# Attention scores of 24 of 32 pair groups as three products of split queries and keys, with two slots for keys, queries and values

## What is computed

```python
scores = scale * np.matmul(q, k.transpose(0, 1, 3, 2))
kth = np.partition(scores, -top_k, axis=-1)[..., -top_k:-top_k + 1]
mask = scores >= kth
scores = np.where(mask, scores, -1000000000.0)
scores = scores - np.max(scores, axis=-1, keepdims=True)
attn = np.exp(scores)
attn = attn / (np.sum(attn, axis=-1, keepdims=True) + 1e-09)
return np.matmul(attn, v).astype(np.float32)
...
h = x @ w_in
g = np.maximum(0.01 * h, h)
return (g @ w_out).astype(np.float32)
...
h = x @ w_in
g = np.where(pos, h, np.where(neg, 0.0, (h + beta) ** 2 / (4.0 * beta)))
return (g @ w_out).astype(np.float32)
```

## Time and profile before

| | |
|---|---|
| median of 3 runs | 1202.42 us (1201.8 to 1202.47) |
| the profiled execution | 1198.35 us |
| its span in the trace | 1196.4 us |
| busy: PE, DVE, ACT, POOL | 1108.2, 924.3, 701.0, 608.7 us |
| DMA queues of SP and ACT, share of 16 engines | 65.5%, 3.9% |

### The profile page before, as it was taken

One profiled execution on the slowest core, in us unless ns is written; L12 is line 12 of the kernel. 1 busy time (PEld: TensorE's weight loads), 2 busy tenths in 40 slices (PEclk: granted clock), 3 DMA queues, 4 the chain that ended last, 5 costly groups with the idle time before them and its releaser, 6 DMA issues.

```text
span 1196.4 us, 21062 instructions
## 1 busy us (share of the span) xinstructions
PE 1108.2 (93%) x7360; PEld 999.2 (84%) x7360; DVE 924.3 (77%) x2088; ACT 701.0 (59%) x1579; POOL 608.7 (51%) x582
## 2 busy tenths in 40 slices
PE   3547998899999999999999989999899999999998
PEld 2335887778989988889987978998789999999998
DVE  7999999989799998998989999969989006300234
ACT  5676878756577765666666756566775424312232
POOL 5676778835366643655536744346644323222222
PEclk9758999989999999999999999999999999999999
DMA  6789997766667787767666756455356677787764
GB/s 228 280 300 342 348 346 285 270 229 206 220 223 233 255 285 257 275 230 258 236 233 211 249 182 222 159 198 175 121 194 217 201 256 250 252 283 251 250 239 150
DMA packets 86792, 287.12 MB, mean 240 GB/s; under 512 B 9632, under 2 KB 13472, under 8 KB 86688
## 3 DMA queue, kind: packets, MB, share of 16 engines
q1 hardware_dynamic: 79200, 270.04, 65.5%
q10 hardware_dynamic: 7488, 15.73, 3.9%
HBM read 247.46 MB, written 38.27 MB: 239 GB/s over the span
## 4 chain that ended last, share of the span: by engine, by line
PE 71%; DVE 19%; POOL 3%; issue 3%; ACT 3%; DMA 1%; POOLq 0%; SPq 0%; ACTq 0%
PE ps_f L812 19%; PE ps_f L820 19%; PE ps_f L813 18%; DVE top L1067 7%; DVE work L1070 7%; PE ps_av L771 6%; PE ps_s L727 3%; PE ps_t L748 2%; DVE drop L1076 2%; PE ps_t L727 2%; DVE part_r L1094 2%; PE ps_t L754 2%; POOL gate L644 1%; POOL drop L630 1%; POOL part_o L650 1%
## 5 line engine op out<-in xcount | busy, mean ns | idle before, releaser
L1067 DVE MAX8 top<-work 128x8 f32<-128x576 f32 x432 | 309.3, 742 | 0.1
L812 PE MATMUL ps_f<-xy,w_ring 128*128 128x384 f32 (+2 forms) x896 | 288.8, 322 | 4.5 <-ACT xy L994 2.5
L820 PE MATMUL ps_f<-gate,w_ring 128*128 128x384 f32 (+2 forms) x896 | 281.3, 314 | 9.5 <-POOL gate L644 9.4
L812 PE MATMUL ps_f<-gate,w_ring 128*128 128x384 f32 (+2 forms) x896 | 286.0, 319 | 1.0 <-ACT part_o L975 0.6
L630 POOL TENSOR_TENSOR drop<-scores,drop 128x576 f32<-128x576 f32 x144 | 207.9, 1444 | 150.1 <-DVE drop L1076 150.1
L820 PE MATMUL ps_f<-xy,w_ring 128*128 128x384 f32 (+2 forms) x896 | 280.8, 313 | 1.8 <-POOL xy L654 1.6
L813 PE MATMUL ps_f<-xy,w_ring 128*128 128x384 f32 (+2 forms) x896 | 280.1, 313 | 0.0
L813 PE MATMUL ps_f<-gate,w_ring 128*128 128x384 f32 (+2 forms) x896 | 280.0, 312 | 0.0
L1070 DVE MATCH_REPLACE8 work<-top,work 128x576 f32<-128x576 f32 x288 | 212.7, 739 | 0.0
L812 PEld LDWEIGHTS ps_f<-xy,w_ring 128*128 128x128 f32 x896 | 169.7, 189 | 20.5 <-issue 9.3
L644 POOL TENSOR_TENSOR gate<-part_r,gate 128x384 fp32r<-128x384 f32 (+2 forms) x112 | 101.5, 909 | 157.4 <-ACT gate L979 157.2
(11 more groups left out here) (83 smaller groups left out, 1822.0 us busy)
## 6 DMA issues: line engine op xcount, KB each, us to landing
w_ring<-w_split SPq DMA_DIRECT2D x412, 512.0 KB, 4.2
w_split<-w_ring SPq DMA_DIRECT2D x36, 512.0 KB, 6.0
raw<-wd SPq DMA_DIRECT2D x64, 256.0 KB, 4.3
w_split<-xy SPq DMA_DIRECT2D x28, 512.0 KB, 3.7
kq<-kqd ACTq DMA_DIRECT2D x12, 576.0 KB, 5.8
v_sb<-vd ACTq DMA_DIRECT2D x12, 320.0 KB, 3.2
out_t<-y_acc ACTq DMA_DIRECT2D x12, 192.0 KB, 3.6
kq<-kqd SPq DMA_DIRECT2D x3, 576.0 KB, 6.7
```

Of the source, the lines that this page charges most:

```text
L812: pe.matmul(out, w[:, 0, m], high, start=first, stop=False)
L820: mm = pe.matmul(out, w[:, 0, m], low, start=False, stop=end)
L1067: dve.max(top[:, t % T_SLOTS, 8 * r:8 * r + 8], source(t, r)).then_inc(dve_step, 1)
```

## The change

**Scores.** For pair groups 8 to 31 (items 20 to 79, 60 of the 80) `kq` is split: ACT copies the loaded queries and keys of the group into `kq_split` high (`high_kq`, one copy of 832 or 960 columns), POOL subtracts for the low part in two halves of 416 or 480 columns (`low_kq`). Both stand three steps before the group's first score, ACT's at the end of the step before. A half of the scores is then three products for each head, float32r each: 12 source instructions an item, one pass each. The first 20 items keep plain float32.

**Mixed items.** They are now written as 128 x 288 products, both heads over 128 stationary columns, where before they were 64 x 64 tiles with a piece of 64 keys apart. For that the host lays out zeros or the first 64 keys again beside queries and keys.

**Loads.** `kq` and `v_sb` have two slots, used by pair group number, and all their loads are issued by SP: 32 groups of keys and queries (the keys of a pair are loaded for both of its groups), 32 of values. SP waits in its own order for the slot: on scores done, on POOL's low part, on values done.

```diff
+KQ_FREE = [score_step(ITEMS[FIRST_OF_GROUP[gp]]) - KQ_AHEAD + 1 if gp >= FIRST_ROUNDED else
+           score_step(ITEMS[LAST_SCORED[gp]]) + 1 for gp in range(GROUPS)]
+KQ_LOAD_AT = {KQ_FREE[gp - KQ_SLOTS]: gp for gp in range(KQ_SLOTS, GROUPS)}
+KQ_LOWERED_AT = {score_step(ITEMS[FIRST_OF_GROUP[gp]]) - KQ_AHEAD: gp for gp in range(FIRST_ROUNDED, GROUPS)}
+V_LOAD_AT = {values_step(gp - V_SLOTS) + 1: gp for gp in range(V_SLOTS, GROUPS)}
...
+            def load_kq(gp):
+                old = gp - KQ_SLOTS
+                if old >= FIRST_ROUNDED:
+                    sp.wait_ge(kq_low_done, 2 * (old - FIRST_ROUNDED + 1))
+                elif old >= 0:
+                    sp.wait_ge(scores_done, 2 * LAST_SCORED[old] + 2)
+                first, end = kq_span(gp)
+                sp.dma_start(kq[:, gp % KQ_SLOTS, first:end], kqd[gp, :, first:end]).then_inc(kq_loaded[gp % KQ_SLOTS], 16)
+            def load_v(gp):
+                if gp >= V_SLOTS:
+                    sp.wait_ge(av_done, gp - V_SLOTS + 1)
...
             for s in range(len(PLAN)):
+                if s in KQ_LOAD_AT:
+                    load_kq(KQ_LOAD_AT[s])
+                if s in V_LOAD_AT:
+                    load_v(V_LOAD_AT[s])
...
+            def low_kq(gp, part):
+                pool.wait_ge(kq_high_done, gp - FIRST_ROUNDED + 1)
+                first, end = kq_parts(gp)[part]
+                slot = kq_split[:, gp % KQ_SLOTS, :, first:end]
+                pool.tensor_tensor(slot[:, 1, :], kq[:, gp % KQ_SLOTS, first:end], slot[:, 0, :].bitcast(F32),
+                                   ALU.subtract).then_inc(kq_low_done, 1)
...
+                if s in KQ_LOWERED_AT:
+                    low_kq(KQ_LOWERED_AT[s], 0)
                 for u in second:
                     event(u)
                 if s in VALUES_AT and s >= READY[0]:
                     low_x(VALUES_AT[s])
                 for u in third:
                     event(u)
+                if s in KQ_LOWERED_AT:
+                    low_kq(KQ_LOWERED_AT[s], 1)
...
+                if it.gp < FIRST_ROUNDED:
+                    exact = kq[:, it.gp % KQ_SLOTS, :]
+                    terms = [(exact, exact)]
+                else:
+                    high, low = kq_split[:, it.gp % KQ_SLOTS, 0, :], kq_split[:, it.gp % KQ_SLOTS, 1, :]
+                    terms = [(high, high), (low, high), (high, low)]
...
+                    even, odd = Q_COLS + j * PART, Q_COLS + j * PART + (REST if it.mixed else 0)
+                    for n, (q, k) in enumerate(terms):
+                        start, stop = n == 0, n == len(terms) - 1
+                        pe.matmul(out[:, 0, 0:PART], q[0:D, rows[0]], k[0:D, even:even + PART], start=start, stop=stop)
+                        mm = pe.matmul(out[:, 1, 0:PART], q[D:P, rows[1]], k[D:P, odd:odd + PART], start=start, stop=stop)
+                    mm.then_inc(scores_done, 1)
...
-                if it.mixed and it.b + 1 < B:
-                    act.dma_start(kq[:, it.pair, :], kqd[(it.b + 1) * PAIRS + it.pair, :, :]).then_inc(kq_loaded[it.pair], 16)
+
+            def high_kq(gp):
+                act.wait_ge(kq_loaded[gp % KQ_SLOTS], 16 * ((gp + 1) // KQ_SLOTS))
+                if gp >= FIRST_ROUNDED + KQ_SLOTS:
+                    act.wait_ge(scores_done, 2 * LAST_SCORED[gp - KQ_SLOTS] + 2)
+                first, end = kq_span(gp)
+                act.activation(kq_split[:, gp % KQ_SLOTS, 0, first:end], kq[:, gp % KQ_SLOTS, first:end], ACT.Copy).then_inc(kq_high_done, 1)
...
-                if gp // PAIRS % 2 and b + 1 < B:
-                    act.dma_start(v_sb[:, pair, :], vd[(b + 1) * PAIRS + pair, :, :]).then_inc(v_loaded[pair], 16)
...
+                if s + 1 in KQ_LOWERED_AT:
+                    high_kq(KQ_LOWERED_AT[s + 1])
```

More of the change, by code:

```diff
@@ L75 @@
 VECTOR_AHEAD = 2
+Q_COLS = 2 * P + REST
+KQ_COLS = Q_COLS + S + REST
+KQ_SLOTS = 2
+V_SLOTS = 2
+KQ_AHEAD = 3
+FIRST_ROUNDED = 8
 S_SLOTS = 4
@@ L425, in sem @@
             return ctx.enter_context(nc.semaphore(name))
[L427 to L428 removed]
+        kq = sb("kq", [P, KQ_SLOTS, KQ_COLS])
+        kq_split = sb("kq_split", [P, KQ_SLOTS, 2, KQ_COLS], F32R)
+        v_sb = sb("v_sb", [P, V_SLOTS, VC])
         scores = sb("scores", [P, S_SLOTS, 2, S])
@@ L461, in build @@
         kq_first = sem("kq_first")
-        kq_loaded = [sem("kq_loaded%d" % p) for p in range(PAIRS)]
-        v_loaded = [sem("v_loaded%d" % p) for p in range(PAIRS)]
+        kq_loaded = [sem("kq_loaded%d" % a) for a in range(KQ_SLOTS)]
+        kq_high_done = sem("kq_high_done")
+        kq_low_done = sem("kq_low_done")
+        v_loaded = [sem("v_loaded%d" % a) for a in range(V_SLOTS)]
         raw_loaded = [sem("raw_loaded%d" % a) for a in range(RAW_SLOTS)]
@@ L716, in score @@
                     pe.wait_ge(kq_first, 32)
-                elif it.rows == 2 or it.rows == 0 and it.gp:
-                    pe.wait_ge(kq_loaded[it.pair], 16 * (it.b + 1))
+                elif it.gp >= FIRST_ROUNDED:
+                    pe.wait_ge(kq_low_done, 2 * (it.gp - FIRST_ROUNDED + 1))
+                elif it.gp and it.n == FIRST_OF_GROUP[it.gp]:
+                    pe.wait_ge(kq_loaded[it.gp % KQ_SLOTS], 16 * ((it.gp + 1) // KQ_SLOTS))
                 need(pe, scores_copied, 2 * it.n)
@@ L721, in score @@
                     need(pe, p_t_copied, ITEMS_OUT[it.n])
-                q, k = kq[:, it.pair, 0:S], kq[:, it.pair, S:2 * S]
-                for j, out in enumerate(score_halves(it)):
[L724 to L736, removed]
-                    pe.matmul(out[0:D, 0, 0:PART], q[0:D, rows], k[0:D, c0:c1],
-                              start=True, stop=True).then_inc(scores_done, 1)
@@ new lines, in score @@
+                if it.gp < FIRST_ROUNDED:
[4 more added lines that the diff above has]
+                    terms = [(high, high), (low, high), (high, low)]
+                first = it.col + Q_COLS - GROUP_WIDTH[it.group]
+                rows = slice(first, first + P), slice(first, first + P)
+                if it.mixed:
+                    rows = rows[0], slice(first + REST - P, first + REST)
@@ L757, in values @@
             def values(gp):
-                b, pair = gp // PAIRS // 2, gp % PAIRS
+                slot = gp % V_SLOTS
                 width = GROUP_WIDTH[gp // PAIRS % 2]
-                pe.wait_ge(v_loaded[pair], 16 * (b + 1))
+                pe.wait_ge(v_loaded[slot], 16 * (gp // V_SLOTS + 1))
                 pe.wait_ge(p_t_copied, ITEM_OF[LAST_OF_GROUP[gp]].n + 1)
@@ L765, in values @@
                         if c < KC:
-                            w = v_sb[:, pair, (a * KC + c) * D:(a * KC + c + 1) * D]
+                            w = v_sb[:, slot, (a * KC + c) * D:(a * KC + c + 1) * D]
                             x = p_t[:, a * KC + c, 0:width]
                         else:
-                            w = v_sb[:, pair, (2 * KC + a) * D:(2 * KC + a + 1) * D]
+                            w = v_sb[:, slot, (2 * KC + a) * D:(2 * KC + a + 1) * D]
                             x = p_rem[:, 0:width]
```

39 lines of the change are left out of this document (22 added, 17 removed).

## The result

The changed kernel takes 1215.25 us (median of 4 runs, 1214.69 to 1216.73) against 1202.11 for the kernel before beside it (4 runs, 1201.74 to 1202.47): ratio 1.0119, 95% interval 1.0104 to 1.0134. It is 1.2% slower. The forecast, 1197.3 us, and its range, 1191 to 1207, both miss it, and the sign is wrong. The profiled execution took 1216.73 us, and that of before lay some 4 us under its kernel's median, so the two spans (1214.9 and 1196.4) differ by 18.5 us and the medians by 13.1.

What follows compares the result with a forecast made beforehand. PE was taken to bound the kernel, except where DVE leads. Saving -8.1, costs +2 and +1 make -5.1: profiled 1198.35 becomes 1193.2, and with the median 4.07 above it, 1197.3 us; range 1191.7 to 1207.

Steps and rivals of the forecast that it cites:

- DVE's own work sets the pace in those steps. I take 0, within 1 us: At the start, moved loads and raw pieces waiting in SP's queue cost nothing, within 1 us to either side.
- a cover for the net's weights: Net weights queued behind SP's key loads: 7.3 us of cover against a wait of at most 6.0, so hidden.
- if the windows before 195 us move: Stated sign that the prediction is wrong: the start, before any changed item is scored, was to stay as it was.
- The added work at the same rate is 1.4 + 0.5 = 2 us: PE's extra waits for POOL's subtractions (1.4) and ACT's copies (0.5), at present waits per busy time: 2 us.
- 1 us for DVE: DVE's find of the dropped slowed by POOL's added work, 0.7 us, with an allowance for the net's square: 1 us.
- 8.1 us: Part of PE's 10.8 us saving on 60 items' scores that reaches the end of the kernel.
- The count by the chain's shares: Items from 195 to 896 us weighted by the net's lines in the chain of waits: 44.8 items at 0.18 us.
- The score block: An item's scores on PE: six float32r pairs, 0.133 us apart, 0.99 us instead of 1.17, saving 0.18 an item.
- (a): PE's score products save nothing, pairs coming every 0.163 us, so only costs stay: 1205 us, chance 0.14.
- (d): The two heads' float32r score products run one behind the other on PE, 37 us more: 1240 us, chance 0.05.
- Rival (c): POOL's first half delays join and low gate, PE losing 1.1 us at half of 24 groups: 1207 us, chance 0.12.
- The signs: Expected in the profile: PE's waits for POOL's gates under 12 us, DVE's for PE's units below 46.8, forecast operation lengths.

Runs made afterwards that it cites:

- e7: Changed kernel with no group split, all scores in plain float32, and SP's key, query and value loads issued last in each step: 1203.42 us.
- e4: e1 with POOL subtracting 16 columns instead of 416 or 480 and PE making three products of high with high: 1199.60 us.
- e1: Changed kernel with SP's loads of keys, queries and values issued behind each step's raw pieces and weight loads: 1206.74 us.
- e13: e5 with its only two splits made of groups 4 and 5, in steps 15 to 18: 1200.37 us.
- e5: e1 with only groups 8 and 9 split, at full width, all 60 items scored from them, SP's later key loads not waiting for POOL: 1201.24 us.
- e8: e1 with POOL's two halves moved just ahead of the masks, in steps 3 and 2 before the first score: 1207.54 us.
- e12: e5 with ACT's copy for group 9, and POOL's halves for it, one step later: 1201.28 us.

## Why the prediction was wrong

By medians, from before to the changed kernel: two slots 1.1 (e7), PE's products with ACT's copies -3.8 (e4 less e7), POOL's low parts 7.1 (e1 less e4), loads ahead 8.5 (changed less e1): together 12.9, measured 13.1. That the sum comes out is no proof of the parts, since each step begins where the one before ends; each part rests on its own pair of kernels, and the short subtractions left in e4 count with PE's.

- **"DVE's own work sets the pace in those steps. I take 0, within 1 us"** (loads at the start) is the step that failed worst: 8.5 us. I looked at who was busy, and not at how much slack the raw pieces had: ACT's wait for them, 22.2 us before 100 us in the trace of before, says that they had none. For the same queue I had worked out a cover for the net's weights, and that was right (PE never waited for `w_ring`); I didn't do it for raw pieces behind the values' load. The text even named the sign, "if the windows before 195 us move". The runs show a queue that stands still up to 6.4 us at a values' load and 7.9 to 8.5 us in the medians.
- **"The added work at the same rate is 1.4 + 0.5 = 2 us"** and 1 us for DVE. For ACT it holds (nothing that the medians show). POOL's low parts cost 7 to 9. The mean rate of waits underrates added work: it comes in lumps of 1.1 to 1.5 us. Where POOL has no gap, a lump arrives whole (2.2 to 2.5 us at tile 30 for two halves), and a chain of DVE, POOL and ACT that is late lengthens a wait that PE has anyway (0.85 to 2.37 us around step 68). How the 7 us divide among such places is read from two executions and is no more than likely. The find of the dropped goes from 564 ns in the mean to 612, 7 us in 144 of them, in place of my 0.7; but in e1 it is 597 and in e4 592, so POOL's low parts make only 0.7 us of it. Most of that increase isn't the length of POOL's subtractions, and what it is stays open.
- **"8.1 us"** of 10.8 should have been 3 to 5 (e13), or 2.2 (e5, with two splits in steps 32 to 37). The count by the chain's shares knew nothing of the clock, and no term of the sum did: by the windows above, PE is at half clock for some 22 us more than before.
- **The score block** (0.18 us less an item, pairs 0.133) is right to 0.01 us, and rivals (a) and (d) are refuted. The rate of 81 ns a matmul that the Trainium skill ("TensorE: Matmul & The Clock Gate", Back-to-back issue gap) gives does not hold for these pairs either: two matmuls every 0.133 us are 67 ns each.
- **Rival (c)**, slower by POOL's first half, had the right kind, POOL's lumps, and 1207 us, which is where e1 stands. That the numbers meet is partly luck: it took 13 us for POOL and 8 for the saving, and the runs have 7 and 4. e8 speaks against the first half's place as the cause.
- **The signs** mostly came true and didn't tell: PE's waits for POOL's gates are 10.1 us from 195 to 896 us (under 12), DVE's for PE's units 44.3 (under 46.8), and the operations have their forecast lengths. Only the windows before 195 us told.

What the last runs leave open: why the 1.7 us at tile 42 that e12 wins are lost again behind step 82, and why the same wait is followed by half the clock in one kernel and not in another. Per group I can't say which of POOL's subtractions costs what.

## What to carry to other kernels

When a load that waits for a slot goes into a queue in order, look at everything behind it, in every phase of the program, and ask of each how long its reader waits already: a reader that waits for DMAs now, as ACT did here for 22.2 us, may have no slack, whatever engine is the busiest. A queue's blocking wait belongs behind the loads that nothing holds up. An engine with a third of its time free may still have none at the few places where the first engine waits for it, so price added work by those waits and by what follows them, not by its share. A saving on the busiest engine arrived here by a fifth to a half (2.2 to 5.4 of 10.8 us), and by 57% of the next 32 us.

## What I had not expected of the hardware

- A wait of PE of some 2 us in the middle of dense work can cost more than itself. Behind waits of 2.33 and 2.37 us the granted clock was 0.72 over 6 us, at 1.2 GHz for more than half of them, and 1.00 behind one of 0.85. But behind the same wait of 2.25 us it was 1.00 in e7 and 0.72 in e13. The Trainium skill ("TensorE: Matmul & The Clock Gate", Part 1: The HAM clock gate) says that one kernel meets a different number of slow matmuls from run to run at its start. No row here shows the start so; these rows show something like it between two kernels, in the middle of work that is already at full clock.
- Two float32r products with 64 rows each, on different rows of the array, run side by side like plain float32 ones: a pair of 288 columns every 0.133 us, where the net's single matmuls over all rows take 0.12 us at 256 columns and 0.15 at 320.
